# Attention and two gated feed-forward layers on one core: ScalarE alone empties the down products, GpSimd and VectorE work in another order between groups, and in attention the two copies of an output half move behind two steps' exponentials

## Chip, cores, metric

The kernel runs on one core of one Trainium2 chip. The metric is the device time of one execution in microseconds (us); the median of three runs of the kernel before is 798.59 us (798.53 to 802.11).

## What is computed

Inputs are float32: `q`, `k`, `v` of 2 batches x 8 heads x 768 x 64, `proj` of 64 x 6, and the weights of two layers. Cut to what matters:

```python
q_bits = (q @ proj > 0); k_bits = (k @ proj > 0)          # 6 bits a row: its bucket
scores = where(q_bucket == k_bucket, q @ k.T / sqrt(64), -1e9)
attn = softmax(scores) @ v                                 # 16 heads
x = attn.transpose(0, 2, 1, 3).reshape(1536, 512)
x = (sigmoid(x @ w_gate) * (x @ w_val)) @ w_out            # d_ff 1536
h = x @ w_in                                               # d_ff 2048
g = where(h >= 1, h, where(h <= -1, 0, (h + 1) ** 2 / 4))
out = g @ w_out2
```

## The kernel before

Every engine has its own program, written out in order; semaphores tie them together. Each float32 operand is split into a high part and a rest, and each product is three matmuls (high x high, high x rest, rest x high).

**Attention** runs in 96 steps `g`, one for 128 rows of queries of a head; 12 steps (`u` = 0 to 11) make a pair of heads `i`, 6 a head, and 3 an output half `j`. In step g TensorE multiplies scores g (L702, L705), turns the probabilities of step g-5 (L714, six transposes) and adds a third of the weighting by v into output half j (`weigh`, L731 and L732; j = (g-8)//3, bank 6 or 7 of PSUM by the parity of j). VectorE evacuates scores g with their minimum (L1200), and subtracts the high part of the turned probabilities (L1211). ScalarE casts the turned probabilities (L907) and takes the exponential (L911). GpSimd normalises (L491). An output half, once complete, is emptied by two copies of 64 rows on ScalarE: `copy_half` to `x` (L918) and `copy_other` to `o_part` (L930), which raises `o_copied`; GpSimd then adds the two (`add_half`, L599). Before, both copies belong to step g = 3j + 11: `copy_half` ahead of the cast, `copy_other` behind the exponential.

In step u = 3 of pairs 1 to 6 TensorE multiplies the sign products of the next pair's queries (`signs`, first matmul L678). They are written to bank 7, where the odd output halves lie, and so wait until `o_copied` has counted the half before:

```python
                if i > 1 and not keys:
                    pe.wait_ge(o_copied, 4 * (i - 1) - 2)
```

For the signs made in step g = 12i + 3 this is output half j = 4i - 3, whose `copy_other` stands in step 12i + 2 of ScalarE's program before.

**The layers** run in 40 sets n: 24 of the first layer (even ones widen the gate, odd ones the value) and 16 hinge sets of the second. A set is seven products (L748 to L750) into two banks in turn; `empty(n, r)` on VectorE (L1276, L1269) empties product r and so frees its bank for product r+2 (product 0 is emptied by ScalarE's `first_product`, L988). Between the products lie `down` units, which multiply finished tiles of the hidden layer by the narrowing weights (L778, L779, L789 to L791); how many stand behind each product is the table `units`. A tile is rounded by ScalarE (L980) and its rest taken by VectorE (`rest_tile`, L1280), which a unit waits for. Batches change at the sets in `FIRSTS` = 0, 12, 24, 32: ahead of one, the next operand is rounded (L943 on ScalarE, `rest_x`, L1222, on VectorE), and in it the six banks of the finished down product are emptied (`empty_y`). GpSimd sums the weight blocks of a set (L504 to L511) and takes their rests (L516 to L522) after ScalarE has rounded them (`round_w`, L954 to L957).

## Time and profile before

| | us |
|---|---|
| median of three runs (range) | 798.59 (798.53 to 802.11) |
| the profiled execution | 800.75 |
| its span | 799.0 |
| TensorE busy in the span | 778.3 |
| VectorE / ScalarE / GpSimd busy | 564.7 / 457.1 / 551.4 |

The span runs from the first to the last instruction of the profiled execution; 1.75 us of its time lie around it. Times in rows are us from the span's start. A matmul's duration holds the pipeline's latency, so the pace of TensorE is read from start to start.

### The profile page before, as it was taken

What the parts mean: (1) busy time and instruction counts of PE and PEld (TensorE: products, weight loads), DVE (VectorE), ACT (ScalarE), POOL (GpSimd) and SP (SyncE); (2) the same over time, 40 slices, a digit from 0 to 9 for tenths busy, and PEclk for the clock granted to TensorE, in tenths of its full rate; (3) what the DMA queues carried; (4) which work ended last, traced back from release to release, by engine and by line L of the source; (5) the groups of instructions that cost most, each with busy time, mean ns of one, the idle gap of its engine ahead of it and who ended that gap; (6) DMA issues with size and microseconds to landing.
All of it is one profiled execution on the core that took longest, in us unless ns stands there. A gap on an engine that the chain in (4) does not pass through costs nothing.

```text
span 799.0 us, 12190 instructions
## 1 busy us (share of the span) xinstructions
PE 778.3 (97%) x4403; PEld 718.2 (90%) x4403; DVE 564.7 (71%) x867; ACT 457.1 (57%) x731; POOL 551.4 (69%) x533
## 2 busy tenths in 40 slices
PE   7999999999999999999999999999999999999998
PEld 6899999998979999999899999988999988899996
DVE  5888888887888576446975655597678677666554
ACT  4888988988997424335434334454455464534543
POOL 4667767778889998877885887776657756466420
PEclk9999999999999999999999999999999999999999
DMA  7896586475100212202021221111121111101002
GB/s 146 183 191 138 134 174 139 82 153 119 54 1 27 77 58 79 77 29 79 27 80 54 80 80 53 53 54 54 37 71 53 47 32 69 65 26 53 1 1 79
DMA packets 61930, 60.08 MB, mean 75 GB/s; under 512 B 28384, under 2 KB 51632, under 8 KB 61872
## 3 DMA queue, kind: packets, MB, share of 16 engines
q1 hardware_dynamic: 61712, 59.32, 28.8%
q8 instruction: 35, 0.57, 0.3%
q14 instruction: 23, 0.19, 0.1%
q10 hardware_dynamic: 160, 0.00, 0.0%
HBM read 37.75 MB, written 3.15 MB: 51 GB/s over the span
## 4 chain that ended last, share of the span: by engine, by line
PE 77%; DVE 8%; ACT 6%; issue 5%; POOL 3%; DMA 0%; SPq 0%; POOLq 0%; DVEq 0%; ACTq 0%
PE ps L748 11%; PE ps L749 11%; PE ps L750 11%; PE ps L778 8%; PE ps L789 5%; PE ps L791 5%; PE ps L790 5%; PE ps L779 4%; PE ps L714 4%; ACT ph L907 2%; PE ps L731 2%; PE ps L732 2%; PE ps L702 2%; DVE probs L1200 2%; PE ps L705 2%
## 5 line engine op out<-in xcount | busy, mean ns | idle before, releaser
L748 PE MATMUL ps<-xop,wset 128*128 128x384 f32 x560 | 191.2, 341 | 5.0 <-DVE u L1276 3.9
L749 PE MATMUL ps<-xop,wset 128*128 128x384 f32 x560 | 189.5, 338 | 0.0
L750 PE MATMUL ps<-xop,wset 128*128 128x384 f32 x560 | 189.0, 338 | 0.0
L1276 DVE TENSOR_TENSOR u<-ps,u 128x384 f32<-128x384 f32 x144 | 79.5, 552 | 102.0 <-PE ps L750 101.8
L516 POOL TENSOR_TENSOR wset<-stage,wset 128x512 fp32r<-128x512 f32 x39 | 54.3, 1392 | 122.0 <-ACT wset L955 122.0
L748 PEld LDWEIGHTS ps<-xop,wset 128*128 128x128 f32 x560 | 105.4, 188 | 20.2 <-issue 8.2
L1211 DVE TENSOR_TENSOR pl<-ps,ph 128x768 fp32r<-128x768 f32 x96 | 91.4, 954 | 26.5 <-ACT ph L907 25.4
L749 PEld LDWEIGHTS ps<-xop,wset 128*128 128x128 f32 x560 | 105.5, 188 | 3.8
L491 POOL TENSOR_SCALAR probs<-probs,small 128x768 f32<-128x768 f32 x96 | 88.3, 927 | 24.9 <-DVE small L1205 22.1
L750 PEld LDWEIGHTS ps<-xop,wset 128*128 128x128 f32 x560 | 105.4, 188 | 0.0
L522 POOL TENSOR_TENSOR wset<-wsum,wset 128x1024 fp32r<-128x1024 f32 x39 | 97.1, 2489 | 0.0
L1200 DVE TENSOR_SCALAR_CACHE_REDUCE probs<-ps 128x768 f32<-128x768 f32 x96 | 90.9, 949 | 5.2 <-PE ps L705 4.6
L911 ACT ACTIVATE probs<-probs,small 128x768 f32<-128x768 f32 x96 | 90.0, 937 | 7.7 <-DVE probs L1200 7.4
L907 ACT CAST ph<-ps 128x768 fp32r<-128x768 f32 x96 | 76.7, 800 | 21.4 <-PE ps L714 19.9
L1276 DVE TENSOR_TENSOR hid<-ps,u 128x384 f32<-128x384 f32 x84 | 46.6, 555 | 51.1 <-PE ps L750 49.5
L714 PE MATMUL ps<-ident,probs 128*128 128x128 f32 x576 | 78.9, 273 | 2.1 <-DVE probs L1200 1.2
L789 PE MATMUL ps<-wo,hh 128*128 128x512 f32 x192 | 75.4, 393 | 4.2 <-DVE hl L1280 4.2
L791 PE MATMUL ps<-wo,hl 128*128 128x512 f32 x192 | 75.5, 393 | 0.0
L790 PE MATMUL ps<-wo,hh 128*128 128x512 f32 x192 | 75.5, 393 | 0.0
L714 PEld LDWEIGHTS ps<-ident,probs 128*128 128x128 f32 x576 | 67.2, 140 | 8.9 <-issue 3.8
L778 PE MATMUL ps<-hh,wo 128*128 128x512 f32 x192 | 75.2, 396 | 0.0
L999 ACT ACTIVATE hid<-hid,small 128x768 f32<-128x768 f32 x32 | 30.0, 937 | 77.4 <-DVE tmp L1307 77.4
(137 smaller groups left out, 1721.7 us busy)
## 6 DMA issues: line engine op xcount, KB each, us to landing
stage<-in_moe_w_in_dram SPq DMA_DIRECT2D x16, 512.0 KB, 3.4
stage<-in_moe_w_out_dram SPq DMA_DIRECT2D x14, 512.0 KB, 4.0
stage<-in_moe_w_gate_dram SPq DMA_DIRECT2D x12, 512.0 KB, 4.3
stage<-in_moe_w_val_dram SPq DMA_DIRECT2D x12, 512.0 KB, 3.6
ops<-qh SPq DMA_DIRECT2D x15, 384.0 KB, 5.3
ops<-kh SPq DMA_DIRECT2D x28, 192.0 KB, 5.1
qn<-in_q_dram SPq DMA_DIRECT2D x16, 192.0 KB, 4.5
kn<-in_k_dram SPq DMA_DIRECT2D x16, 192.0 KB, 5.0
```

What stands on the lines that cost most here:

```text
L522: pool.tensor_tensor(weights(n, 1)[:, 3:7], wsum[:, :], weights(n, 0)[:, 3:7].bitcast(F32), ALU.subtract).then_inc(w_split, 1)
L714: last = pe.transpose(dst[:, t * P:(t + 1) * P], probs[n % RING][:, t * P:(t + 1) * P], ident[:, :])
L748: pe.matmul(dst, high[:, c, :], high_x(r)[:, c, :], start=(c == 0), stop=False)
L749: pe.matmul(dst, high[:, c, :], low_x(r)[:, c, :], start=False, stop=False)
L750: last = pe.matmul(dst, low[:, c, :], high_x(r)[:, c, :], start=False, stop=(c == 1))
L778: pe.matmul(main, w[:, cols], h[:, t % 3, 0:512], start=(first and n == 0), stop=(last_tile and n == 2))
L789: pe.matmul(ps[:, r, :], hh[:, t % 3, rows], wh, start=first, stop=False)
L790: pe.matmul(ps[:, r, :], hh[:, t % 3, rows], wl, start=False, stop=False)
L791: last = pe.matmul(ps[:, r, :], hl[:, t % 3, rows], wh, start=False, stop=last_tile)
L907: act.copy(dst, turned_slot("T", n).rearrange("p (t n) -> p t n", t=T)).then_inc(pt_high, 1)
L1200: dve.tensor_scalar(probs[g % RING].rearrange("p (s n) -> p s n", s=2), score_slot(g), NO_MATCH, None, ALU.min, ALU.min, accum_out=lowest( ...
L1276: dve.tensor_tensor(dst, bank(n, r), other, ALU.add).then_inc(e_dve, 1)
```

## The change

It does four things. (1) In attention `copy_half` stands behind the exponential of step 3j + 11 and `copy_other` behind that of step 3j + 12; GpSimd's `add_half` and `first_sum` move by one step. (2) `empty_y` is ScalarE's alone, with semaphore `emptied_y`; the weights of the set behind a first set are rounded in the first set, not ahead of it, and GpSimd starts on them when all rests of the new operand are taken. (3) In value sets away from a first set VectorE empties product 6 ahead of the gating of the second tile. (4) Around first hinge sets VectorE's, ScalarE's and TensorE's orders change.

```diff
-                if g % HT == 0 and 12 <= g < STEPS:
-                    add_half((g - 12) // HT, g - HT + 1)
+                if g % HT == 1 and 13 <= g < STEPS:
+                    add_half((g - 13) // HT, g - HT + 1)
...
-                    pool.wait_ge(hl_ready, 2 * pair_of(n - 2) + 2)
+                    pool.wait_ge(x_low, R * (group_of(n) + 1))
...
                 if n in (N1 + 1, FIRSTS[3] + 1):
-                    return (0, 0, 1, 1, 2, 2, 2)[r]
+                    return (0, 0, 0, 0, 2, 2, 4)[r]
...
             def empty_y(g):
 
                 if g < 2:
                     act.wait_ge(tile_used, T1 * (g + 1))
-                    act.copy(x[:, g, 0:2, 0:512], ps[:, 0:2, :])
-                    act.copy(x[:, g, 0:2, 512:S], ps[:, 4, :].rearrange("p (c n) -> p c n", c=2)).then_inc(y_act, 1)
+                    act.copy(x[:, g, :, 0:512], ps[:, 0:KT, :])
+                    act.copy(x[:, g, :, 512:S], ps[:, 4:6, :].rearrange("p a (c n) -> p (a c) n", c=2)).then_inc(emptied_y, 1)
...
             def gate_set(n):
                 pp, g = pair_of(n), group_of(n)
                 first_product(n)
                 if n in FIRSTS:
+                    round_w(n + 1)
                     empty_y(g - 1)
...
             def hinge_set(n):
                 t, g = 2 * pair_of(n), group_of(n)
                 ahead = n + 1 in FIRSTS
-                first_product(n)
+                if n - 1 not in FIRSTS:
+                    first_product(n)
                 if n in FIRSTS:
+                    round_w(n + 1)
                     empty_y(g - 1)
-                    hinge_part(t)
+
+                    hinge_relu(t)
+                    first_product(n + 1)
+                    hinge_square(t)
                     return
...
             for g in range(STEPS):
                 i, u = g // U, g % U
-                if g % HT == 2 and g >= 11:
-                    copy_half((g - 11) // HT)
                 if g >= LAG:
                     high_probs(g - LAG)
...
                 exponential(g)
                 if g % HT == 2 and g >= 11:
-                    copy_other((g - 11) // HT)
+                    copy_half((g - 11) // HT)
+                if g % HT == 0 and g >= 12:
+                    copy_other((g - 12) // HT)
...
                 empty(n, 5)
-                gate_second(n)
-                empty(n, 6)
+                if n - 1 in FIRSTS or n + 1 in FIRSTS:
+
+                    gate_second(n)
+                    empty(n, 6)
+                else:
+                    empty(n, 6)
+                    gate_second(n)
                 gate_first(n)
...
                 if n in FIRSTS:
-                    empty_y(g - 1)
+                    empty(n + 1, 1)
                 add_hinge(t)
                 clamp(t + 1)
                 if ahead:
                     rest_tile(t)
+                    sum_x(g + 1, 3)
+                    add_hinge(t + 1)
                     rest_x(g + 1, 2)
-                    add_hinge(t + 1)
-                    rest_x(g + 1, 3)
                     rest_tile(t + 1)
-                    for r in MADE[4:]:
+                    for r in MADE[3:]:
                         rest_x(g + 1, r)
```

ScalarE's program in attention, before, from the exponential of the second step of a pair (u = 1) to the cast in u = 4 (`ph` the cast, `probs` the exponential, `x` copy_half, `o_part` copy_other):

```order
L911 ACTIVATE probs,small<-probs,small 128x768 [waits evacuated]
L918 COPY x<-ps 64x384 [waits o_ready]
L907 CAST ph<-ps 128x6x128 [waits o_ready,pt_ready]
L911 ACTIVATE probs,small<-probs,small 128x768 [waits evacuated]
L930 COPY o_part<-ps 64x384 [waits o_done]
L907 CAST ph<-ps 128x6x128 [waits pt_ready]
L911 ACTIVATE probs,small<-probs,small 128x768 [waits evacuated]
L907 CAST ph<-ps 128x6x128 [waits pt_ready]
```

and of the change:

```order
L910 ACTIVATE probs,small<-probs,small 128x768 [waits evacuated]
L906 CAST ph<-ps 128x6x128 [waits o_ready,pt_ready]
L910 ACTIVATE probs,small<-probs,small 128x768 [waits evacuated]
L917 COPY x<-ps 64x384 [waits o_ready]
L906 CAST ph<-ps 128x6x128 [waits pt_ready]
L910 ACTIVATE probs,small<-probs,small 128x768 [waits evacuated]
L929 COPY o_part<-ps 64x384 [waits o_done]
L906 CAST ph<-ps 128x6x128 [waits pt_ready]
```

`o_part` stood ahead of the cast of step u = 3; now the cast and the exponential of that step stand ahead of it. TensorE's program has the same rows here in both: its sign products of step u = 3 wait for `o_copied`, which `o_part` raises.

VectorE's program at the end of a value set in the middle of a group, before (`tmp` is product 5, `u` product 6, `hid<-hid,tmp` and `hid<-hid,u` the gating, the last `u` product 1 of the next set):

```order
L1276 TENSOR_TENSOR tmp<-ps,u 128x384 [waits p_done]
L1295 TENSOR_TENSOR hid<-hid,tmp 128x768 [waits e_dve]
L1276 TENSOR_TENSOR u<-ps,u 128x384 [waits e_dve,p_done]
L1300 TENSOR_TENSOR hid<-hid,u 128x384 [waits e_dve]
L1276 TENSOR_TENSOR u<-ps,u 128x384 [waits e_dve,gated,e_act,p_done]
```

and of the change:

```order
L1283 TENSOR_TENSOR tmp<-ps,u 128x384 [waits p_done]
L1283 TENSOR_TENSOR u<-ps,u 128x384 [waits e_dve,p_done]
L1302 TENSOR_TENSOR hid<-hid,tmp 128x768 [waits e_dve]
L1307 TENSOR_TENSOR hid<-hid,u 128x384 [waits e_dve]
L1283 TENSOR_TENSOR u<-ps,u 128x384 [waits e_dve,gated,e_act,p_done]
```

The emptying of product 6 now stands ahead of the first gating.

VectorE's program in the first hinge set, before, from the clamp of its first tile on (`x<-ps` is empty_y, `hl` the rest of a tile):

```order
L1307 TENSOR_SCALAR tmp<-hid 128x768 [waits e_dve]
L1276 TENSOR_TENSOR hid<-ps,u 128x384 [waits e_dve,p_done]
L1316 COPY x<-ps 128x2x512 [waits tile_used]
L1317 COPY x<-ps 128x2x256
L1311 TENSOR_TENSOR hid<-hid,tmp 128x768 [waits hinge_parts]
L1307 TENSOR_SCALAR tmp<-hid 128x768 [waits hinge_done,e_dve]
L1276 TENSOR_TENSOR u<-ps,u 128x384 [waits e_dve,e_act,p_done]
L1280 TENSOR_TENSOR hl<-hid,hh 128x768 [waits hh_ready]
```

and of the change:

```order
L1314 TENSOR_SCALAR tmp<-hid 128x768 [waits e_dve]
L1283 TENSOR_TENSOR hid<-ps,u 128x384 [waits e_dve,p_done]
L1283 TENSOR_TENSOR u<-ps,u 128x384 [waits e_dve,e_act,p_done]
L1318 TENSOR_TENSOR hid<-hid,tmp 128x768 [waits hinge_parts]
L1314 TENSOR_SCALAR tmp<-hid 128x768 [waits hinge_done,e_dve]
L1283 TENSOR_TENSOR hid<-ps,u 128x384 [waits hl_ready,p_done]
L1287 TENSOR_TENSOR hl<-hid,hh 128x768 [waits hh_ready]
```

The two copies to `x` are gone, and the emptying of the next set's product 1 (`u`) and product 2 (`hid`) stand ahead of the tile's rest.

## Rows read from the trace of the kernel before

**Rows 1.** The page: engines over the whole span, and TensorE's granted clock in 40 slices.

```profile
PE 778.3 (97%) x4403; PEld 718.2 (90%) x4403; DVE 564.7 (71%) x867; ACT 457.1 (57%) x731; POOL 551.4 (69%) x533
PEclk9999999999999999999999999999999999999999
```

**Rows 2.** Timeline, ScalarE, pair 4, steps u = 2 and 3: start, duration.

```profile
130.10 0.48 ACT L918 COPY x<-ps 64x384 f32<-64x384 f32 x1
130.59 0.80 ACT L907 CAST ph<-ps 128x768 fp32r<-128x768 f32 x1
131.29 0.93 ACT L911 ACTIVATE probs<-probs,small 128x768 f32<-128x768 f32 x1
...
132.21 0.46 ACT L930 COPY o_part<-ps 64x384 f32<-64x384 f32 x1
...
133.28 0.94 ACT L911 ACTIVATE probs<-probs,small 128x768 f32<-128x768 f32 x1
```

**Rows 3.** Timeline, TensorE: scores and signs of u = 3 in pair 4.

```profile
130.92 0.51 PE L702 MATMUL ps<-ops 128*128 128x384 f32 x2
...
132.98 0.34 PE L678 MATMUL ps<-qh,wq_h 128*128 128x384 f32 x1
```

**Rows 4.** Timeline, TensorE: first and last of six such signs.

```profile
45.90 0.34 PE L678 MATMUL ps<-qh,wq_h 128*128 128x384 f32 x1
...
192.16 0.34 PE L678 MATMUL ps<-qh,wq_h 128*128 128x384 f32 x1
```

**Rows 5.** Timeline, VectorE: evacuation of the scores of u = 3.

```profile
132.29 0.95 DVE L1200 TENSOR_SCALAR_CACHE_REDUCE probs<-ps 128x768 f32<-128x768 f32 x1
```

**Rows 6.** Timeline, ScalarE's casts three steps apart; TensorE's scores of two steps.

```profile
111.94 0.80 ACT L907 CAST ph<-ps 128x768 fp32r<-128x768 f32 x1
...
118.43 0.80 ACT L907 CAST ph<-ps 128x768 fp32r<-128x768 f32 x1
...
118.52 0.51 PE L702 MATMUL ps<-ops 128*128 128x384 f32 x2
...
120.58 0.51 PE L702 MATMUL ps<-ops 128*128 128x384 f32 x2
```

**Rows 7.** Timeline, end of value sets; in brackets idle time before, and releaser.

```profile
288.62 1.47 DVE L1295 TENSOR_TENSOR hid<-hid,tmp 128x768 f32<-128x768 f32 x1
290.00 0.55 DVE L1276 TENSOR_TENSOR u<-ps,u 128x384 f32<-128x384 f32 x1
...
290.70 0.41 PE L748 MATMUL ps<-xop,wset 128*128 128x384 f32 x1 [0.62 <-DVE u L1276]
...
435.08 0.41 PE L748 MATMUL ps<-xop,wset 128*128 128x384 f32 x1 [0.16 <-DVE u L1276]
```

**Rows 8.** Timeline, first hinge sets, VectorE and TensorE.

```profile
545.42 1.21 DVE L1316 COPY x<-ps 128x1024 f32<-128x1024 f32 x1
...
549.14 0.95 DVE L1280 TENSOR_TENSOR hl<-hid,hh 128x768 fp32r<-128x768 f32 x1
...
547.25 0.45 PE L748 MATMUL ps<-xop,wset 128*128 128x384 f32 x1 [0.27 <-ACT u L988]
...
550.15 0.78 PE L789 MATMUL ps<-wo,hh 128*128 128x512 f32 x1 [1.56 <-DVE hl L1280]
```

**Rows 9.** Stretches: length, busy time of PE, PEld, DVE, ACT, POOL, then granted clock.

```profile
550.20:553.60 3.40, 3.40 (x10) 3.12 (x11) 1.43 (x2) 2.37 (x5) 0.21 (x1) 0.50 0.01 2
...
681.00:682.00 1.00, 0.89 (x4) 0.76 (x5) 0.44 (x2) 0.59 (x1) 0.00 (x0) 1.00 0.01 0
```

**Rows 10.** Timeline, TensorE at the last change of batch.

```profile
659.58 0.50 PE L789 MATMUL ps<-wo,hh 128*128 128x512 f32 x1 [1.06 <-DVE hl L1280]
...
681.11 0.50 PE L789 MATMUL ps<-wo,hh 128*128 128x512 f32 x1 [1.54 <-DVE hl L1280]
```

**Rows 11.** Timeline, VectorE's rests without and with GpSimd at work.

```profile
526.77 0.95 DVE L1222 TENSOR_TENSOR xop<-x,xop 128x768 fp32r<-128x768 f32 x1
...
532.21 1.49 DVE L1222 TENSOR_TENSOR xop<-xt,xop 128x768 fp32r<-128x768 f32 x1
```

More of the change, by code:

```diff
@@ L336, in build @@
         hh_ready, hl_ready, tile_used = sem("hh_ready"), sem("hl_ready"), sem("tile_used")
-        y_act, y_dve = sem("y_act"), sem("y_dve")
+        emptied_y = sem("emptied_y")
         bank_ready = sem("bank_ready")
@@ L448, in _ @@
                 if n == FIRSTS[3] + 3:
-                    for half, ready in ((0, y_act), (HT, y_dve)):
-                        sp.wait_ge(ready, 3)
+                    sp.wait_ge(emptied_y, 3)
+                    for half in (0, HT):
                         sp.dma_start(out_v[0, :, half:half + HT, :], osb[:, half:half + HT, :]).then_inc(stored, 16)
@@ L628, in _ @@
                     first_set(i - 1)
-                if i == NP - 3 and u in (4, 7, 10):
-                    first_sum(0 if u == 4 else 2, (u - 7) // 3)
-                if i == NP - 2 and u in (4, 7, 10):
-                    first_sum(1 if u == 4 else 3, (u - 7) // 3)
+                if i == NP - 3 and u in (3, 6, 9):
+                    first_sum(0 if u == 3 else 2, (u - 6) // 3)
+                if i == NP - 2 and u in (3, 6, 9):
+                    first_sum(1 if u == 3 else 3, (u - 6) // 3)
                 if i == NP - 1 and u % 3 == 1:
@@ L760, in tile_waits @@
                 if g and t in (T1, TILES1, TILES1 + T2):
-                    pe.wait_ge(y_act, g)
-                    pe.wait_ge(y_dve, g)
+                    pe.wait_ge(emptied_y, g)
             def down1(t, c):
@@ L938, in round_x @@
                     elif g > 1:
-                        act.wait_ge(y_act, g - 1)
-                        act.wait_ge(y_dve, g - 1)
+                        act.wait_ge(emptied_y, g - 1)
                 elif r == 1:
@@ L994, in sigmoids, with hinge_relu, hinge_square @@
                     act.activation(hidden(pp, second), hidden(pp, second), ACT.Sigmoid).then_inc(sig_done, 1)
+            def hinge_relu(t):
+                act.wait_ge(clamped, t - TILES1 + 1)
+                act.activation(tile(t), tile(t), ACT.Relu, bias=minus_one).then_inc(hinge_parts, 1)
+            def hinge_square(t):
+                act.activation(tmp[:, :], tmp[:, :], ACT.Square, bias=half, scale=0.5).then_inc(hinge_parts, 1)
             def hinge_part(t):
-                m = t - TILES1
-                act.wait_ge(clamped, m + 1)
-                act.activation(tile(t), tile(t), ACT.Relu, bias=minus_one).then_inc(hinge_parts, 1)
-                act.activation(tmp[:, :], tmp[:, :], ACT.Square, bias=half, scale=0.5).then_inc(hinge_parts, 1)
+                hinge_relu(t)
+                hinge_square(t)
             def empty_y(g):
@@ L1010, in empty_y @@
                     act.wait_ge(x_low, 4 * R)
-                    act.copy(osb[:, 0:HT, :], ps[:, 0:HT, :]).then_inc(y_act, 1)
+                    act.copy(osb, ps[:, 0:T, :]).then_inc(emptied_y, 1)
             def gate_set(n):
@@ L1046, in value_set @@
                         round_wo2(n)
-                    round_w(n + 2)
             def hinge_set(n):
@@ L1051, in hinge_set @@
                 ahead = n + 1 in FIRSTS
-                first_product(n)
+                if n - 1 not in FIRSTS:
+                    first_product(n)
                 if n in FIRSTS:
+                    round_w(n + 1)
                     empty_y(g - 1)
-                    hinge_part(t)
+                    hinge_relu(t)
+                    first_product(n + 1)
+                    hinge_square(t)
                     return
@@ L1076, in hinge_set @@
                     round_x(g + 1, 5)
-                    round_w(n + 2)
             act.dma_start(projn[0:D, :], proj).then_inc(proj_in, 16)
@@ L1106, in _ @@
                     round_x(0, u - 1)
+            copy_other(2 * NH - 4)
             high_probs(STEPS - 5)
@@ L1230, in sum_x @@
                     if g > 1:
-                        dve.wait_ge(y_act, g - 1)
-                        dve.wait_ge(y_dve, g - 1)
+                        dve.wait_ge(emptied_y, g - 1)
                     dve.tensor_tensor(xt[:, 0], b22, b12, ALU.subtract).then_inc(x_sums, 1)
@@ L1342, in gate_set @@
                 empty(n, 6)
-                if n in FIRSTS:
-                    empty_y(g - 1)
             def value_set(n):
@@ L1369, in hinge_set @@
                 ahead = n + 1 in FIRSTS
-                empty(n, 1)
-                if n not in FIRSTS:
+                if n - 1 not in FIRSTS:
+                    empty(n, 1)
+                if n - 1 in FIRSTS:
+                    empty(n, 2)
                     rest_tile(t - 2)
+                    empty(n, 3)
                     add_hinge(t - 1)
-                empty(n, 2)
-                empty(n, 3)
-                if n not in FIRSTS:
-                    rest_tile(t - 1)
+                else:
+                    if n not in FIRSTS:
+                        rest_tile(t - 2)
+                        add_hinge(t - 1)
+                    empty(n, 2)
+                    empty(n, 3)
+                    if n not in FIRSTS:
+                        rest_tile(t - 1)
                 if ahead:
@@ L1380, in hinge_set @@
                 empty(n, 4)
-                if ahead:
-                    rest_x(g + 1, 1)
+                if n - 1 in FIRSTS:
+                    rest_tile(t - 1)
                 sum_ahead(n)
@@ L1386, in hinge_set @@
                 if ahead:
-                    sum_x(g + 1, 3)
+                    rest_x(g + 1, 1)
                 empty(n, 6)
                 if n in FIRSTS:
-                    empty_y(g - 1)
+                    empty(n + 1, 1)
                 add_hinge(t)
```

10 lines of the change are left out of this document (removed).

## The prediction

> **What bounds the kernel now.** I read the page first: TensorE is busy 778.3 of 799.0 us and its clock is granted in full in all but a few us [rows 1]. So whatever is won or lost is a wait of TensorE, and 799.0 - 778.3 = 20.7 us (a little more by start to start, since busy time holds the pipeline's tails) is all that could be won. Then I went through the timeline of TensorE and looked, wherever two starts lie further apart than the work between them, at what released it. In attention there is almost no such place: a plain step takes 120.58 - 118.52 = 2.06 us of pure issue, three take 6.2, while ScalarE's casts come every 118.43 - 111.94 = 6.49 us [rows 6], so ScalarE, coupled with VectorE, costs TensorE 0.3 us per three steps in part of each pair of heads, and nothing where sign products and turns give TensorE more work. In the layers the waits stand at the ends of value sets [rows 7] and at the changes of batch [rows 8, 10].
>
> **Attention: one wait appears, six times.** The sign products of u = 3 begin at 132.98, 2.06 us behind their step's first scores at 130.92 [rows 3]: TensorE reaches them with no wait, for the o_part copy they need began at 132.21 and took 0.46 [rows 2], so that it ended 0.31 us early. In the change that copy stands behind the exponential of the same step u = 3. This exponential can't be early: it needs the scores that TensorE issued at 130.92 and VectorE's evacuation of them, which starts at 132.29 [rows 5]; it began at 133.28. The copy followed its exponential after 132.21 - 131.29 = 0.92 us. So the new copy begins at 133.28 + 0.92 = 134.20, ends at 134.66, and the sign product starts some 0.12 later (an estimate: VectorE's end at 290.55 to TensorE's start at 290.70 is 0.15 [rows 7]): 134.78 against 132.98, a wait of 1.8 us. The other copy moves too: its 130.59 - 130.10 = 0.49 us lay ahead of the cast at 130.59 and now lies between the exponential of u = 2 and the next cast. The exponential of u = 3 then starts at 131.29 + 1.05 + 0.49 + 0.70 = 133.53 (1.05 an estimate, the 0.93 of the exponential and its accumulator's read; 0.70 is 131.29 - 130.59), 0.25 later. That gives 2.05; I take 2.1, since the step of the turned queries (u = 0) now holds a copy more on ScalarE as well. Bounds: 1.6 if the cast at 130.59 comes forward by 0.2, 2.4 if ScalarE is late by another 0.3.
>
> Behind the waiting product on TensorE stand the scores and turns of u = 4; VectorE, ScalarE and GpSimd all live on these, so nothing uses the wait and all later steps shift by it. It comes once a pair for six pairs, first at 45.90 and last at 192.16 [rows 4]: 6 x 2.1 = **+12.6** (9.6 to 14.4).
>
> What spreading the copies wins: before, the loop cast, VectorE's rest, evacuation, exponential, copy, cast, exponential, copy takes the 6.49 us. In the new order another cast starts the same loop, with the same two copies in it. The round is as long, only shifted by a step. I take 0; the upper bound is 0.3 us for two rounds in each of seven pairs, -4. GpSimd's add_half only changes places with a normalisation: 0.
>
> **The clock.** A wait this long can cost twice. Behind the wait of 1.56 us at 550.15 [rows 8] the granted clock was 0.50, that is 1.2 GHz, over 3.4 us [rows 9], and the matmuls of that stretch came 1.6 us late in all (an estimate: 3.4 us at half pace lose 1.7, and the idle matmuls' ends give a little back). Behind a wait of 1.54 us at 681.11 [rows 10] the clock stayed at 1.00 [rows 9]. Of two equal waits one cost a fall, and the new ones are longer than both; so between none and six falls, 0 to +9.6. I take two, **+3.2**.
>
> **Value sets.** The gating of the second tile took 1.47 us from 288.62, product 6 was emptied only at 290.00, and TensorE waited for it at 290.70 [rows 7], 0.62 idle. Its idle time began at 290.70 - 0.62 = 290.08, at the end of product 0 of the next set; that is six matmuls, each of which adds 0.51 - 0.34 = 0.17 us [rows 3], so product 6 had ended at 290.08 - 1.04 = 289.04. With the emptying first its bank is free at 289.04 + 0.55 = 289.6, before TensorE wants it at about 289.95. Now the gating is late by 0.5 us instead: the next in line are ScalarE's casts of the tile and the next set's product 1, whose emptying must end by 292.0; I get 291.9 to 292.1, a wait of 0.1. So 0.6 is won in each of four sets of the first group, and 0.25 in each of four of the second (0.16 idle at 435.08 [rows 7], and 0.09 of a weight load that starts late, an estimate): 2.4 + 1.0, **-3.4** (-1.5 to -4).
>
> **Changes of batch.** At 550.15 TensorE waited 1.56 us for a tile's rest, after 0.27 at 547.25 [rows 8], then ran at half clock. The rest at 549.14 was late through VectorE's two copies, which begin at 545.42, the first with 1.21 us, the second of half the columns. They go to ScalarE, which takes some 3 us for all six banks (double the columns, an estimate) while it waits for the clamp anyway. The down units also wait until product 4. By these two the rest would be ready in time, but the next obstacle is product 4's bank: VectorE must first do add_hinge, a clamp and the emptying of product 2, which keeps TensorE for 0.7 (quiet GpSimd) to 1.4 us (busy). Won: 1.8 + 1.6 of clock - 0.9 = 2.5. The same at 681.11, without a fall: 1.54 + 0.2 - 0.7 = 1.0, and at 659.58 the 1.06 idle [rows 10] disappears, since the emptying of product 6 and the tile's rest come ahead of an addition: with the restart, 1.2. Add 0.3 at the first change. Sum 5.0, I round to **-5.3** with the small waits for ScalarE's first_product (-2.5 to -7).
>
> GpSimd's start on the next set's weights now lies behind all rests. VectorE's rests took 0.95 us before GpSimd started and 1.49 beside it [rows 11], so six of them end about 3 us sooner, and GpSimd's block behind them, some 8 us (an estimate), still ends about 1.3 us before TensorE wants the weights. It costs 0; if that cover goes, a wait of up to 1 us at each of three changes.
>
> The Trainium skill (SBUF - State Buffer, Who interferes with whom) speaks against this step: a VectorE instruction with two SBUF inputs contends with a reading GpSimd instruction, and whichever issues first holds the shared ports for its whole length. By that rule GpSimd's block, moved into the first hinge set, would block each two-input instruction there, and the gain at this change would go. The trace agrees that they slow each other, with the 1.49 for 0.95.
>
> **The sum.** Against the profiled execution, 800.75 us (span 799.0 and 1.75 around it): 800.75 + 12.6 + 3.2 - 3.4 - 5.3 = 807.85. That execution lies 2.2 us above the median of 798.59, of which 1.6 is the fall of the clock at 550, already taken out in the sum; for the remaining 0.6 I take off as much: 807.25, **807.2 us**, 1.1% above the median.
>
> **Rivals.**
> (A) Mine, with one to four falls of the clock: 807.2 - 1.6 = 805.6 to 807.2 + 3.2 = 810.4. Chance 0.50.
> (B) The clock holds behind all six waits, as it did at 681.11: 807.2 - 3.2 = 804.0. Speaks for it that attention shows 1.00 throughout; against, the length. 0.20.
> (C) It falls behind five or six: 812.0 to 813.6. 0.08.
> (D) The wait of the signs is only 1.2 us: the chain of scores 0.7, evacuation 0.95, exponential 0.93, copy 0.46 [rows 2, 3, 5] and 0.2 for the handovers is 3.2 us when no engine is late, less the 2.06 that passes anyway. Six are 7.2 and no fall follows: 804.0 - (12.6 - 7.2) = 798.6, no difference. It needs VectorE to start on the scores at once; at 132.29 it started 0.7 us after them. 0.12.
> (E) The other sign: the copy for the signs is in time after all, because ScalarE runs ahead once its copies lie in two steps; no wait, no fall, and rounds of 6.2 instead of 6.49: 807.2 - 12.6 - 3.2 - 4 = 787.4. It decides from the exponential of u = 3 being done by 132.4, while its scores are evacuated only from 132.29. 0.04.
> (F) GpSimd's block spoils the first hinge set: 5 two-input instructions of VectorE x (1.49 - 0.95) = 2.7 us at one change [rows 11], GpSimd's sums and rests of the next set lying beside VectorE's additions and rests; with my waits and falls 807.2 + 2.7 = 809.9. 0.06. The rule cited above from the Trainium skill (SBUF - State Buffer) would bring this about.
>
> **Range and chances.** Between B's lower edge and C: 800.5 to 812 leaves out E, half of D and most of C. Half a per cent of 798.59 is 4 us, about what a measurement of this kernel can tell from no change: 802.6 and above is slower. A, C, F and most of B lie there: 0.80. Same: most of D and a little of B, 0.15. Faster: 0.05.
>
> **What would show it.** In the changed profile: six sign products whose matmul is released by ScalarE's o_part copy with 1.9 us idle, at intervals of about 31 instead of 29 us; granted clock of 0.50 behind some of them; ScalarE's casts still 6.5 us apart elsewhere; no wait of more than 0.2 us at the ends of middle value sets; at the first hinge sets a wait for VectorE's `hid` at product 4 in place of the one for `hl`. I am wrong if the signs start 2.1 us behind their scores, if the clock falls at all six, or if TensorE waits for GpSimd's weights at sets 13, 25 or 33.

## The result and the profile after

The changed kernel takes 805.66 us (median of six, 805.54 to 807.26). The kernel before takes 798.81 us beside it (six, 798.45 to 802.11). The ratio is 1.008, with a 95% interval of 1.0062 to 1.0098: slower by 0.9%. The prediction was 807.2, range 800.5 to 812, slower with 0.80.

The profiled execution took 807.26 us, with a span of 805.1. The page of the changed kernel, engines and granted clock; its counterpart is [rows 1]:

```profile
span 805.1 us, 12180 instructions
...
PE 776.7 (96%) x4403; PEld 718.3 (89%) x4403; DVE 552.6 (69%) x862; ACT 462.3 (57%) x731; POOL 537.6 (67%) x533
...
PEclk9999999999999999999999999999999999999999
```

TensorE has the same 4403 matmuls and is busy 1.6 us less, in a span 6.1 us longer. So all of the loss is time in which TensorE stands idle. The view of waits of the changed kernel, TensorE alone (waiting line, releaser: total us, times, longest), names the largest of it:

```profile
PE ps L678 <- ACT o_part L929: 10.5, 6, 1.8
PE ps L731 <- issue: 2.1, 8, 0.4
PE ps L748 <- DVE u L1283: 1.8, 7, 0.4
PE ps L748 <- DVE hid L1283: 1.8, 3, 0.9
```

The first row is the wait that the prediction put at the centre: six times, for the `o_part` copy. Neither it nor a wait of a weighing (the second row) was in attention before. In turn a small wait of before is gone, that of the turning of the next pair's queries (L665) in the same view of the kernel before:

```profile
PE ps L665 <- DVE pl L1211: 1.3, 5, 0.3
```

The timeline of the large wait, its first, second, fourth and last time:

```profile
48.87 0.41 PE L678 MATMUL ps<-qh,wq_h 128*128 128x384 f32 x1 [1.75 <-ACT o_part L929]
...
80.14 0.42 PE L678 MATMUL ps<-qh,wq_h 128*128 128x384 f32 x1 [1.76 <-ACT o_part L929]
...
142.67 0.42 PE L678 MATMUL ps<-qh,wq_h 128*128 128x384 f32 x1 [1.75 <-ACT o_part L929]
...
206.05 0.42 PE L678 MATMUL ps<-qh,wq_h 128*128 128x384 f32 x1 [1.76 <-ACT o_part L929]
```

Two such products now lie 80.14 - 48.87 = 31.27 us apart; before, the third lay 103.95 - 74.92 = 29.03 behind the second. The last of the five intervals is 0.8 to 1.1 longer in every kernel, so that the six of before, from 45.90 to 192.16 [rows 4], are (192.16 - 45.90) / 5 = 29.25 apart on the mean. From first to last the changed kernel needs 157.18 us and the kernel before 146.26: 10.92 more in five intervals, 2.18 each.

What releases the product at 142.67 stands in the same timeline on TensorE, VectorE and ScalarE. It is to be held against [rows 2, 3, 5]:

```profile
138.70 0.51 PE L702 MATMUL ps<-ops 128*128 128x384 f32 x2
...
139.91 0.95 DVE L1208 TENSOR_SCALAR_CACHE_REDUCE probs<-ps 128x768 f32<-128x768 f32 x1
...
139.95 0.48 ACT L917 COPY x<-ps 64x384 f32<-64x384 f32 x1
140.44 0.80 ACT L906 CAST ph<-ps 128x768 fp32r<-128x768 f32 x1
141.13 0.94 ACT L910 ACTIVATE probs<-probs,small 128x768 f32<-128x768 f32 x1
...
142.06 0.46 ACT L929 COPY o_part<-ps 64x384 f32<-64x384 f32 x1
```

The scores of the step begin at 138.70, their evacuation at 139.91, and the exponential at 141.13. The copy starts 142.06 - 141.13 = 0.93 behind the exponential, and the sign product 142.67 - 142.06 = 0.61 behind the copy. The product starts 3.97 us behind its scores, where before it was 132.98 - 130.92 = 2.06 [rows 3]. The difference is 1.91.

The second row of the waits is one weighing in each of six pairs and two more in the last. The same timeline around one of them, on ScalarE, VectorE and TensorE:

```profile
121.21 0.47 ACT L929 COPY o_part<-ps 64x384 f32<-64x384 f32 x1
121.71 0.80 ACT L906 CAST ph<-ps 128x768 fp32r<-128x768 f32 x1
...
122.54 0.96 DVE L1219 TENSOR_TENSOR pl<-ps,ph 128x768 fp32r<-128x768 f32 x1 [0.43 <-ACT ph L906]
...
123.60 0.41 PE L731 MATMUL ps<-ph,v 128*128 128x384 f32 x1 [0.26 <-issue]
```

The cast begins as the copy ends, VectorE waits for the cast, and the weighing starts 123.60 - 123.50 = 0.10 behind VectorE's rest (122.54 + 0.96). The trace calls the releaser "issue"; by the order in time and the program, whose weighing waits for this rest, it is the rest.

The clock did not fall behind any of the six: the granted clock was 1.00 in the 3.4 us behind each. Stretches of the changed kernel behind a sign product and behind the longest wait in the layers (length, busy time of the five, granted clock, and two columns of DMA):

```profile
142.60:146.00 3.40, 3.33 (x21) 3.33 (x22) 0.97 (x2) 0.63 (x1) 2.15 (x3) 1.00 1.07 243
561.60:565.00 3.40, 3.36 (x17) 3.13 (x18) 3.40 (x6) 2.38 (x4) 0.11 (x1) 1.00 0.19 68
```

The layers got faster, as this table of the timelines shows. Each number is the time from the first product (L748) of one set to that of another, in us; "value sets alone" and "batch alone" are the experiments below.

| stretch (sets) | before | changed | value sets alone | batch alone |
|---|---|---|---|---|
| 2 to 11 | 108.59 | 106.92 | 106.96 | 108.59 |
| 12 to 13, first change of batch | 8.17 | 7.75 | 8.17 | 7.77 |
| 14 to 22 | 94.82 | 94.07 | 94.15 | 94.89 |
| 22 to 24 | 32.50 | 31.98 | 31.98 | 32.55 |
| 25 to 26, first hinge set | 16.81 | 14.58 | 16.79 | 14.58 |
| 31 to 32, last rests | 28.59 | 27.30 | 28.59 | 27.31 |
| 33 to 34, first set of the last batch | 15.15 | 13.64 | 16.71 | 13.66 |

From the start of set 0 to the end, the kernel before takes 799.0 - 242.81 = 556.19 us and the changed one 805.1 - 256.91 = 548.19, 8.0 less. Of that, 1.6 is the fall of the clock which the profile of before happens to hold at 550 [rows 9]: in the profile of the second experiment, whose layers are those of before, sets 25 to 26 took 15.22 us instead of 16.81, without a fall. Set 0 itself starts 14.1 later, and 14.1 - 8.0 = 6.1 is the difference of the spans.

What now ends the idle times in the sets behind the two first hinge sets, in the timeline of TensorE:

```profile
561.64 0.45 PE L748 MATMUL ps<-xop,wset 128*128 128x384 f32 x1 [0.91 <-DVE hid L1283]
...
688.31 0.44 PE L748 MATMUL ps<-xop,wset 128*128 128x384 f32 x1 [0.56 <-DVE hid L1283]
```

They answer to the 1.56 of [rows 8] and the 1.54 of [rows 10]. Elsewhere ScalarE's casts lie as far apart as before: three steps in 128.20 - 121.71 = 6.49 us.

### The profile page after: what moved, and what is told of

Its sections match the earlier page's. It is cut to its first block, busy times and chain, and to the rows that moved or that the text cites. A ratio compares the mean times of both kernels' runs of the same rounds, so it can differ in the third digit from the quotient of the medians.

```text
span 805.1 us, 12180 instructions
## 1 busy us (share of the span) xinstructions
PE 776.7 (96%) x4403; PEld 718.3 (89%) x4403; DVE 552.6 (69%) x862; ACT 462.3 (57%) x731; POOL 537.6 (67%) x533
## 4 chain that ended last, share of the span: by engine, by line
PE 81%; DVE 6%; ACT 6%; POOL 3%; issue 3%; DMA 0%; SPq 0%; DVEq 0%; POOLq 0%; ACTq 0%
PE ps L748 12%; PE ps L749 11%; PE ps L750 11%; PE ps L777 8%; PE ps L789 5%; PE ps L790 5%; PE ps L788 5%; PE ps L714 5%; PE ps L778 4%; PE ps L702 3%; PE ps L731 3%; PE ps L705 3%; PE ps L732 2%; ACT probs L910 2%; ACT ph L906 2%
## 5 line engine op out<-in xcount | busy, mean ns | idle before, releaser
L748 PE MATMUL ps<-xop,wset 128*128 128x384 f32 x560 | 191.0, 341 | 4.3 <-DVE u L1283 1.8
L516 POOL TENSOR_TENSOR wset<-stage,wset 128x512 fp32r<-128x512 f32 x39 | 56.5, 1448 | 114.2 <-ACT wset L953 114.2
L748 PEld LDWEIGHTS ps<-xop,wset 128*128 128x128 f32 x560 | 105.2, 188 | 18.4 <-issue 3.8
L522 POOL TENSOR_TENSOR wset<-wsum,wset 128x1024 fp32r<-128x1024 f32 x39 | 95.3, 2444 | 0.0
L731 PE MATMUL ps<-ph,v 128*128 128x384 f32 x192 | 72.3, 376 | 2.8 <-issue 2.1
```

Source lines behind the costliest of these rows:

```text
L522: pool.tensor_tensor(weights(n, 1)[:, 3:7], wsum[:, :], weights(n, 0)[:, 3:7].bitcast(F32), ALU.subtract).then_inc(w_split, 1)
L731: pe.matmul(o_bank(j), v2[h % 2][:, t, :], ph[j % 2][:, t, :], start=(t == 0), stop=False)
L748: pe.matmul(dst, high[:, c, :], high_x(r)[:, c, :], start=(c == 0), stop=False)
```

## The experiments

Medians and ranges are in us. "Before" is the kernel before on the same chip.

**1. The changed kernel with attention as before.** My theory puts all of the loss into attention.

```diff
 # in the changed kernel, ScalarE
+                if g % HT == 2 and g >= 11:
+                    copy_half((g - 11) // HT)
                 if g >= LAG:
                     high_probs(g - LAG)
...
                 if g % HT == 2 and g >= 11:
-                    copy_half((g - 11) // HT)
-                if g % HT == 0 and g >= 12:
-                    copy_other((g - 12) // HT)
+                    copy_other((g - 11) // HT)
```

GpSimd's `add_half` and `first_sum` go back a step with it, and the last `copy_other`, which the change has behind the loop, goes back into it.

> The changed kernel with the attention part as it was before (both copies in step 3j + 11, add_half and first_sum at their old steps); all edits of the layers stay. Wait theory (the six waits of the sign products, some 2.2 us a pair, are all that the change costs): 805.7 - 13.1 = 792.5 us, with no wait for o_part and the pairs 29.0 us apart. Rival (the changed attention part is dear through more than these waits, or the layers' edits depend on it): above 795 or below 790.

791.99 (791.84 to 792.28, five) against 798.64; ratio 0.9912 (0.9898 to 0.9926). The layers' edits alone make the kernel faster by 6.65 us, and undoing the attention part is worth 13.7 against the changed kernel. The plain intervals of its sign products are 29.0 us.

**2. The kernel before with the new attention alone.** The same edit the other way.

> The kernel before with the attention part of the change alone. Wait theory: 798.8 + 13.1 = 812 us, six waits of 1.75 us for o_part, and 0 to 6 falls of the granted clock behind them at up to 1.6 us each; the changed kernel's profile showed none. Rival (the layers' edits win nothing by themselves, the profile before was only slow there): 806 us.

811.98 (811.86 to 816.84, five), ratio 1.0177 (1.0153 to 1.0202): +13.3. The two halves add up: 13.3 - 6.65 = +6.7, and the changed kernel measured 805.66 - 798.81 = +6.85. The view of waits of this kernel and its timeline:

```profile
PE ps L678 <- ACT o_part L930: 10.5, 6, 1.8
...
PE ps L731 <- issue: 2.2, 8, 0.4
```
```profile
47.01 0.41 PE L678 MATMUL ps<-qh,wq_h 128*128 128x384 f32 x1 [1.75 <-ACT o_part L930]
...
78.27 0.41 PE L678 MATMUL ps<-qh,wq_h 128*128 128x384 f32 x1 [1.76 <-ACT o_part L930]
```

These are the same six waits at the same spacing, with 2.2 us of waits at the weighing. Nothing of the loss comes from the layers. Two of the five runs were slower than the rest, 813.93 and 816.84, at a mean granted clock of 0.998 and 0.996; no profile shows where it fell in them.

**3. One copy early.** This tests whether the six waits are the loss, or the new places of the copies as such. Only the `copy_other` that the signs wait for returns to its step.

```diff
 # in the changed kernel, ScalarE
                 if g % HT == 2 and g >= 11:
                     copy_half((g - 11) // HT)
+                    if (g - 11) // HT % 4 == 1:
+                        copy_other((g - 11) // HT)
-                if g % HT == 0 and g >= 12:
+                if g % HT == 0 and g >= 12 and (g - 12) // HT % 4 != 1:
                     copy_other((g - 12) // HT)
```

> The changed kernel, but for one output half in four (j % 4 == 1, those that the sign products wait for) copy_other stands in step 3j + 11 again, behind copy_half, both behind the exponential; the others stay spread over two steps. Wait theory: 792 to 794 us, since the copy is done some 0.3 us around the time TensorE comes; a wait of up to 0.5 us may stay, for copy_half now stands ahead of it behind the same exponential. Rival (the new places of all the copies cost, through the loop of ScalarE and VectorE): 798 us or more, with the 0.25 us waits of weigh and the pairs 30 us apart.

795.97 (795.47 to 796.57, five), ratio 0.9961 (0.9948 to 0.9975). The wait is gone but for 0.15 us in one place, yet the kernel stays 4.0 slower than the first experiment and above the 792 to 794 expected, without reaching the 798 of the rival. Its timeline:

```profile
75.04 0.41 PE L678 MATMUL ps<-qh,wq_h 128*128 128x384 f32 x1 [0.15 <-ACT o_part L929]
...
104.68 0.41 PE L678 MATMUL ps<-qh,wq_h 128*128 128x384 f32 x1
...
116.89 0.41 PE L731 MATMUL ps<-ph,v 128*128 128x384 f32 x1 [0.26 <-issue]
```

An interval of 104.68 - 75.04 = 29.64 us is 0.6 more than the 29.0 of the first experiment. In this kernel ScalarE has both copies in one step again for those halves, both behind the exponential, so it is not a clean measure of the copies' places, and it does not say how its 4.0 us divide. The next one is cleaner.

**4. The signs a step later.** All copies stay where the change puts them. TensorE's sign products of the queries move from u = 3 to u = 4, ahead of those of the keys.

```diff
 # in the changed kernel, TensorE
-                if u == late(i) + 3 and i < NP - 1:
-                    signs(i + 1, False)
                 if u == late(i) + 4 and i < NP - 1:
+                    signs(i + 1, False)
                     signs(i + 1, True)
```

> The changed kernel, but TensorE makes the sign products of the queries in step u = 4, next to those of the keys, and not in u = 3. Nothing is left out. It comes to them 2.05 us later and the copy takes no part in the wait: wait theory 792 to 794 us, no idle of TensorE before the first sign product. If the cost sits in the copies' order on ScalarE and not in this wait: 798 us or more, as in the rival of the run before. It may cost a little that the sign products lie together (2.1 us in which ScalarE and VectorE get nothing new): up to 1 us a pair, 798, which the idle times would show on ScalarE and not as a wait of TensorE for o_part.

793.87 (793.49 to 794.46, five), ratio 0.9934 (0.9921 to 0.9947). No sign product waits for `o_part`, and they lie 106.19 - 76.94 = 29.25 us apart:

```profile
76.94 0.34 PE L678 MATMUL ps<-qh,wq_h 128*128 128x384 f32 x1
...
106.19 0.34 PE L678 MATMUL ps<-qh,wq_h 128*128 128x384 f32 x1
...
116.22 0.41 PE L731 MATMUL ps<-ph,v 128*128 128x384 f32 x1 [0.25 <-issue]
```

This splits the 2.24 us by which a plain interval grew, from 29.03 to 31.27: 31.27 - 29.25 = 2.02 is the wait, and 0.22 is what the copies' new places add, which nothing in the prediction held. It is a balance. The step in which the weighing waits lasts 2.53 us from scores to scores (143.70 to 146.23, L702), where in the first experiment it lasts 2.16 (142.57 to 144.73), and the other steps of the pair, among them the one whose wait at the turned queries is gone, give a part of these 0.37 back. Six waits are 12.1 us. The whole kernel is 793.87 - 791.99 = 1.9 us slower than the first experiment; the signs' own later place is in this number too, and no run parts the two.

**5. `copy_other` alone.** The kernel before, with `copy_other` (and GpSimd's additions) a step later, and `copy_half` where it was.

```diff
 # in the kernel before, ScalarE
                 exponential(g)
-                if g % HT == 2 and g >= 11:
-                    copy_other((g - 11) // HT)
+                if g % HT == 0 and g >= 12:
+                    copy_other((g - 12) // HT)
```

> The kernel before, with copy_other alone a step later (add_half and first_sum with it, as in the change); copy_half stays ahead of the cast of step 3j + 11. Part of the sum that is put on copy_other: the six waits of 1.8 us and no more, 798.6 + 10.8 = 809.4 us; and 0.25 us a pair less than with copy_half moved as well (812.0). Rival: the loop of ScalarE and VectorE sets the time whatever stands in it, and it is 812.0 as well.

810.77 (810.31 to 812.03, four) against 800.38 (798.6 to 800.9, 21 runs), ratio 1.0144 (1.013 to 1.0158). The lowest runs differ by 11.7, between the 10.8 of the wait alone and the 13.4 of the rival. The waits are a little shorter, and the products lie 109.14 - 78.14 = 31.0 apart:

```profile
78.14 0.42 PE L678 MATMUL ps<-qh,wq_h 128*128 128x384 f32 x1 [1.70 <-ACT o_part L930]
...
109.14 0.42 PE L678 MATMUL ps<-qh,wq_h 128*128 128x384 f32 x1 [1.68 <-ACT o_part L930]
```

So one moved copy makes the wait. The move of `copy_half` adds the rest, 31.27 - 31.0 = 0.27 a pair; with `copy_half` in its old place the weighing of a pair does not wait.

**6. A longer wait.** To find out whether such a wait can make the clock fall at all: three further copies on ScalarE ahead of each `o_part` copy that the signs wait for, and ahead of a seventh one, in the last pair, for which no signs wait. They write to unused memory, and nothing is left out.

```diff
 # in the changed kernel, ScalarE
+            def fill(j):
+                for _ in range(3):
+                    if filled_n[0]:
+                        act.wait_ge(filled, filled_n[0])
+                    act.copy(spare[0:D, :], o_bank(j)[0:D, :]).then_inc(filled, 1)
+                    filled_n[0] += 1
...
                 if g % HT == 0 and g >= 12:
+                    if (g - 12) // HT % 4 == 1:
+                        fill((g - 12) // HT)
                     copy_other((g - 12) // HT)
```

> The changed kernel with three more copies of 64 x 384 on ScalarE (of the output half, to memory that nothing reads) ahead of the six copies for which the sign products wait. Each waits for the one before. They take 0.5 to 0.65 us each, so the wait of TensorE goes from 1.75 to 3.3 to 3.7 us. If the whole added time of ScalarE reaches the path: 805.7 + 6 x 1.5 to 1.9 = 814.7 to 817 us with the clock at 1.00. If waits of this length do make the granted clock fall where those of 1.75 did not: up to 1.6 us more each, 817 to 826. If ScalarE catches up part of it elsewhere: below 814.

824.56 (824.36 to 825.84, four), ratio 1.0313 (1.0296 to 1.033). The timeline of this kernel, then its stretches behind two of the waits:

```profile
48.83 0.41 PE L679 MATMUL ps<-qh,wq_h 128*128 128x384 f32 x1 [3.14 <-ACT o_part L939]
...
83.05 0.41 PE L679 MATMUL ps<-qh,wq_h 128*128 128x384 f32 x1 [3.14 <-ACT o_part L939]
```
```profile
48.80:52.20 3.40, 3.37 (x13) 3.30 (x14) 0.25 (x1) 0.00 (x0) 1.91 (x2) 0.58 1.17 204
82.80:86.20 3.40, 3.15 (x12) 3.09 (x13) 0.00 (x0) 0.10 (x1) 1.91 (x2) 0.60 1.05 241
```

In 3.4 us there are 12 or 13 matmuls instead of 21. The clock fell behind all six: the granted clock was 0.55 to 0.58 in the 3.4 us behind each. The spacing is 83.05 - 48.83 = 34.22, that is 2.95 over the 31.27. Of it 3.14 - 1.75 = 1.39 is the wait itself, and the remaining 1.56 is the price of one fall, the 1.6 that the prediction had taken from [rows 9]. A seventh, shorter fall stood behind a wait of 1.60 for a rest, ahead of the first set. This wait is the work of the seventh group of fill copies, which hold the cast ahead of the rest:

```profile
255.85 0.41 PE L732 MATMUL ps<-ph,v 128*128 128x384 f32 x1 [1.60 <-DVE pl L1231]
```
```profile
255.80:259.20 3.40, 2.93 (x15) 2.68 (x15) 3.40 (x5) 1.94 (x4) 2.15 (x3) 0.76 0.01 2
```

Six times 2.95 is 17.7, of the 824.56 - 805.66 = 18.9 measured. From the last sign product to set 0 this kernel takes 274.39 - 220.61 = 53.78 us and the changed one 256.91 - 206.05 = 50.86; of these 2.92, 1.56 are the sixth fall and the remaining 1.4 the seventh group. The mean granted clock of this run is 0.985 with seven falls, some 0.002 for each.

**7. The order in value sets alone**, in the kernel before.

```diff
 # in the kernel before, VectorE
                 empty(n, 5)
-                gate_second(n)
-                empty(n, 6)
+                if n - 1 in FIRSTS or n + 1 in FIRSTS:
+                    gate_second(n)
+                    empty(n, 6)
+                else:
+                    empty(n, 6)
+                    gate_second(n)
                 gate_first(n)
```

> The kernel before, with only the order in value sets of the change (product 6 emptied ahead of the gating, in the eight sets away from a first set). By the traces of before and after, sets 2 to 11 took 108.59 and 106.92 us and sets 14 to 21 94.82 and 94.07, so 2.4 us in all: 796.2 us. As predicted, 3.4: 795.2. Rival: VectorE was only late in that profile, 798.6.

797.32 (795.59 to 800.64, twelve) against 800.38, ratio 0.9973 (0.996 to 0.9985). The lowest runs differ by 3.0. By the table above it wins 1.63 + 0.67 + 0.52 = 2.8 us, against the 2.4 and 3.4 expected. The profiled execution was the slowest of the twelve, with two falls of the clock, one behind each wait for a tile's rest in a first hinge set:

```profile
548.46 0.50 PE L789 MATMUL ps<-wo,hh 128*128 128x512 f32 x1 [1.91 <-DVE hl L1280]
...
679.42 0.56 PE L789 MATMUL ps<-wo,hh 128*128 128x512 f32 x1 [1.52 <-DVE hl L1280]
```
```profile
549.60:553.00 3.40, 3.40 (x13) 3.11 (x12) 2.22 (x4) 3.04 (x6) 1.30 (x1) 0.56 0.01 2
680.00:682.50 2.50, 2.50 (x8) 2.31 (x8) 1.36 (x2) 1.57 (x4) 0.00 (x0) 0.50 0.00 0
```

The second is the place at which the kernel before had waited 1.54 us without a fall [rows 9, 10]; sets 33 to 34 took 16.71 us here against 15.15, 1.56 more. The mean granted clock of this run was 0.996.

**8. The changes of batch alone**: the first experiment's kernel with the value sets' old order.

```diff
 # in the kernel of the first experiment, VectorE
-                if n - 1 in FIRSTS or n + 1 in FIRSTS:
-                    gate_second(n)
-                    empty(n, 6)
-                else:
-                    empty(n, 6)
-                    gate_second(n)
+                gate_second(n)
+                empty(n, 6)
```

> The attention part and the value sets as before; only the edits around the changes of batch (ScalarE empties the down product alone, GpSimd's wait, the orders in the sets next to a first one, the units table). From the 792.0 us of the kernel with all edits of the layers, less what the value sets give: 794.4 us (2.4) to 795.4 (3.4). Rival, that the two kinds of edits do not add up: outside 794 to 796.

795.98 (795.12 to 799.33, ten), ratio 0.9959 (0.9946 to 0.9972), above the 794.4 to 795.4 expected; the kernel before has 800.38 on this chip, 1.7 above the 798.64 that this sum started from. The lowest runs differ by 3.5. In the table it wins 0.40 + 2.23 + 1.28 + 1.49 = 5.4 us, of which 1.6 is the fall of the clock in the profile of before. The value sets keep their waits (TensorE's timeline of this kernel):

```profile
339.04 0.41 PE L748 MATMUL ps<-xop,wset 128*128 128x384 f32 x1 [0.50 <-DVE u L1282]
```

By the lowest runs 3.0 + 3.5 = 6.5 us, and both together, in the first experiment, gave 6.5 by the lowest runs too. The parts add up.

**9. GpSimd's start as before**, in the first experiment's kernel. It is the only edit to which the prediction gave 0 while a rule spoke against it.

```diff
 # in the kernel of the first experiment, GpSimd
-                    pool.wait_ge(x_low, R * (group_of(n) + 1))
+                    pool.wait_ge(hl_ready, 2 * pair_of(n - 2) + 2)
```

> The kernel with attention as before and all edits of the layers (792.0 us), but GpSimd starts on the next set's weights as before, when the last tile's rest is taken and not when all rests of the operand are. If GpSimd beside VectorE is what made the rests slow (1.49 for 0.95 us) and this reached TensorE: 793 us, with the rests at 1.49 us again. If the first hinge sets then have a quiet GpSimd sooner, as the rule on the shared ports would have it: 791.5. If it lies off the path: 792.0 within 0.3.

792.55 (792.45 to 792.92, four). That is 0.56 above the first experiment's 791.99, more than the 0.3 allowed for, but on another chip, and below the 792.98 of its repeat. VectorE's rests beside GpSimd take 1.49 us again (528.78), where they take 0.95 (527.38) in the first experiment, and GpSimd's sums 1.45 (526.59) instead of 0.74 (531.71). Yet TensorE waits 0.90 us at 546.93 for `hid` where the first experiment has 0.91, and the stretches of the table agree within 0.05 (22 to 24 apart, 0.2). The two engines do slow each other, and it does not reach TensorE: the place of this wait moves nothing that can be told from the spread between chips.

**10. Product 2 first.** The prediction named VectorE's emptying of product 2 as the next obstacle in a first hinge set. Here it goes ahead of the second clamp.

```diff
 # in the kernel of the first experiment, VectorE
                 if n - 1 in FIRSTS:
-                    empty(n, 2)
                     rest_tile(t - 2)
...
                 add_hinge(t)
+                if n in FIRSTS:
+                    empty(n + 1, 2)
                 clamp(t + 1)
```

> The kernel with attention as before and all edits of the layers, and in the sets behind a first hinge set VectorE empties product 2 ahead of the clamp of the second tile, not behind it. The wait of TensorE for it was 0.9 us at one change of batch and 0.56 at the other. If it is that emptying's place alone: 792.0 - 1.4 = 790.6 us, and waits under 0.1. If the tile's rest is then late instead and TensorE waits for it at the down unit: 791.5 to 792.

791.93 (791.58 to 793.28, five), ratio 0.9904 (0.9887 to 0.9921). The wait for product 2 is gone and a wait for the tile's rest stands in its place (TensorE's timeline):

```profile
548.06 0.50 PE L788 MATMUL ps<-wo,hh 128*128 128x512 f32 x1 [0.63 <-DVE hl L1286]
```

This is the second of the two expectations. Sets 25 to 26 took 14.47 instead of 14.54 and 33 to 34 13.30 instead of 13.63. VectorE has no room there (busy 5.86 of the 6.0 us from 544.0); the order chooses which consumer waits. Its median is 1.0 below that of the first experiment's kernel on the same chip, which comes next; but their runs overlap, and the two stretches hold only 0.4 of it.

**The first experiment's kernel again**, on the chip of the sixth and the tenth, for the spread between chips.

> The kernel with attention as before and all edits of the layers once more, to stand beside the run before on the same chip: 792.0 us.

792.98 (791.9 to 793.62, five), before 800.41, ratio 0.9913 (0.9899 to 0.9928). It repeats the ratio of 0.9912. The two profiled executions of this one kernel took 791.84 and 793.62 us, both at a granted clock of 1.00. From the second pair's sign products (21.15 and 22.87) to the end they take 768.55 and 768.53, so the whole difference lies in the first 23 us. There TensorE waited 0.75 us for the first DMA instead of 0.37, and its first turn took 1.54 us instead of 1.17; why was not tried. The best versions are this one and the tenth, near 792: 0.9% under the kernel before and 1.7% under the changed one.

## Why the prediction was right, and where it was not

**The wait of the signs** was right in mechanism, place and count: six sign products, released by the `o_part` copy. It was predicted at 2.1 us and measured at 2.02 (fourth experiment). The idle time in the rows is 1.75, where the prediction had said 1.9. Part of the rest stands right behind the wait: the first product takes 0.41 instead of 0.34 and the next starts 0.60 instead of 0.53 behind it. The chain was worked out from the exponential, that the scores and their evacuation hold back, then the copy behind it. [rows 2, 3, 5] showed all of its members. Rival D, that ScalarE and VectorE would be at their quickest, needed the evacuation to start at once behind the scores; it began 1.21 us behind their first matmul, as against 1.37 before. The wait was not 1.2 us.

**"What spreading the copies wins: 0"** was wrong by a small amount and to the other side. It costs 0.22 us a pair, and up to 1.9 in the whole kernel (fourth experiment). The prediction argued by the length of ScalarE's round, which did stay the same. But a weighing's first part waits for the third of three casts and its rest. In the program before no copy stood ahead of that cast; now `copy_other` stands right ahead of it, and `copy_half` ahead of the one before (the order in the program; the timeline above shows the cast held by the copy). With `copy_other` alone in its new place the weighing of a pair did not wait (fifth experiment), so it takes both.

**The clock: +3.2, measured 0.** This is the term that failed. It took "of two equal waits one cost a fall" as a chance for the six. In the profile of the changed kernel six waits of 1.75 did not make the clock fall, and neither did they in the profiles of the second and fifth experiments (1.65 to 1.76): 18 without a fall. All six runs of the changed kernel had a mean granted clock of 0.999 or 1.0, while two falls gave 0.996 and seven 0.985. At 3.14 all six did fall, at the predicted price. So rival B's mechanism held, whose 804.0 lies 1.7 below the measured time. The measured 805.66 stands at the lower edge of A's 805.6 to 810.4, but not through the falls that A is made of.

**Value sets: -3.4, measured -2.8.** The size is 0.6 off. The gain was counted alike for four sets each; in the first group sets 3 and 5 still wait 0.38 and 0.26 us for product 1 of the next set, where the prediction had said 0.1. By the table the first group won 1.63 to 1.67 instead of 2.4, and the second 1.2 to 1.3 instead of 1.0.

**Changes of batch: -5.3, measured -5.4**, both with the 1.6 of that profile's clock. By piece: first change 0.3 predicted, 0.42 measured; at 550, 2.5 and 2.23; at 659, 1.2 and 1.29; at 681, 1.0 and 1.51. The new waits for `hid`, 0.91 and 0.56, fall in or near the 0.7 to 1.4 given. At 681 0.14 of the surplus is the 0.56 for 0.7; the rest was not taken apart.

**GpSimd's new start: 0** was right (ninth experiment), and rival F with its 809.9 wrong. TensorE did not wait for weights at sets 13, 25 or 33. The two engines do slow each other, 1.49 us for 0.95 [rows 11, ninth experiment]. The Trainium skill (SBUF - State Buffer, Who interferes with whom) states that a VectorE instruction with two SBUF inputs contends with a GpSimd instruction that reads SBUF. The trace agrees as to durations, 1.49 for 0.95 on VectorE and 1.45 for 0.74 on GpSimd. On which side of the rests the block lies changed nothing that TensorE waits for.

**The sum by measured parts**: +12.1 of waits and +1.9 of the copies' places, less the layers' 6.65, is +7.35 against a measured +6.85. The predicted 807.2 is 1.5 too high, and that it is not further off is luck, since errors partly cancel: 3.2 of clock not paid and 0.5 too much for the waits stand against 1.9 of the copies' places and 0.6 of the value sets not foreseen. These make 1.2 of the 1.5; some 0.1 more is the changes of batch, and the rest is not placed.

## What to carry to other kernels

When an operation moves behind another on the same queue, ask what that other one waits for: here a half-microsecond copy moved behind an exponential that could not start until TensorE's next scores were made and evacuated, and the consumer waited some four times the copy's length. Name the consumer of every moved operation by its semaphore, since six of the some thirty moved `o_part` copies carried some 12 of the 13.7 us that attention lost. Edits of unlike places that a change brings together are to be run apart: here a gain of 0.8% lay under a loss of 1.7%.

## What the runs showed of the hardware that was not expected

The clock does not follow the wait's length alone. In attention 18 waits of 1.65 to 1.76 us left the granted clock at 1.00. In the layers waits of 1.91 and 1.52 were followed by 0.56 and 0.50 (seventh experiment), and the kernel before had one of 1.56 followed by 0.50 and one of 1.54 followed by 1.00 [rows 8 to 10]. The second and fifth experiments have the layers of before and waited at the same two places, 1.57 and 1.54 us, and 1.57 and 1.50: all four were followed by 1.00. In the sixth experiment waits of 3.14 in attention were followed by 0.58 and 0.60, and one of 1.60 by 0.76. So the same wait at the same place is followed by a fall in one execution and not in the next, and each fall cost 1.6 us (sets 25 to 26: 16.81 with it, 15.22 and 15.26 without; sets 33 to 34: 16.71 and 15.15). In the times it shows too: where the mean granted clock is listed as 0.998 or less, the kernel before took 800.6 to 800.9 us, and at 0.999 or 1.0 between 798.6 and 800.5 (21 runs on one chip). Some of its runs near 800.4 have a clock of 1.0, so that the clock isn't all of this spread; the two profiles of the first experiment's kernel differ by as much, 1.78 us, in their first 23 us alone. What decides on a fall at a given length, the work before the wait or the moment, was not tried and stays open.
